# A fused attention and two-layer kernel on one core: second group of early weights loaded behind chunk 22, attention rows of chunks 16 to 23 stored after chunk 23

## The chip, the cores and the metric

The kernel runs on one core of one Trainium2 chip. The metric is the device time in microseconds (us) of one execution. Three runs of the kernel before gave 1062.04, 1062.69 and 1062.05 us; the median is 1062.05 us. The profiled execution took 1062.24 us, with a span of 1060.5 us from its first to its last instruction, so 1.7 us lie around the span.

## The reference, cut to what matters

```
# decayed linear attention, 4 batches, 8 heads, 768 positions, head size 64
for t in range(S):
    state = gamma[None, :, None, None] * state + np.einsum('bhd,bhe->bhde', k[:, :, t], v[:, :, t])
    y[:, :, t] = scale * np.einsum('bhd,bhde->bhe', q[:, :, t], state)
x = y.transpose(0, 2, 1, 3).reshape(3072, 512)
# first layer (512 -> 2048 -> 512)
h = np.maximum(x @ w_in, 0.0); x = h * h @ w_out
# second layer (512 -> 1536 -> 512), gated, behind an RMS norm
xn = x / sqrt(mean(x * x) + 1e-06) * rms_g
out = (silu(xn @ w_gate) * (xn @ w_val)) @ w_out2
```

## The kernel before, in words

**Stages.** The kernel is written engine by engine, with explicit semaphores; every engine runs its own list in order. First comes the attention, in 24 chunks of 128 positions (4 batches of 6 chunks). Then come two layers over three token tiles. Every 2x2 block matrix product in them is done with seven block products (a Strassen form), and every factor is split into a high and a low part, so that a product is three matmuls (lines 898 to 900).

**Attention.** The q, k and v rows of a chunk (1 MiB, or 0.75 MiB for the last chunk of a batch) go into one of five places of `qkv_sb`. SyncE's list issues the load of chunk n+5 when chunk n is done (line 473). TensorE does, for a chunk, the scores (line 820, one chunk ahead), the part from the state (line 839), the state's update (line 873) and the masked part (line 849). VectorE masks the scores (line 1389), scales the state (line 1398) and copies the chunk's result out (line 1378). Eight results go straight into `raw`, where the first token tile is made. The other 16 go to DRAM (`x_scratch`), issued from ScalarE's list by `store_x` (line 1003), through three small places of `y_sb` in turn. The results of chunks 18 to 23 are held: those of 18 to 22 are issued in ScalarE's round for chunk 22, and that of 23 in the round for chunk 23. The held results of chunks 21 to 23 lie in freed parts of `qkv_sb`.

**Early weights.** During the attention GpSimd and ScalarE also prepare two groups ("quads") of the first layer's second weights. A quad is 1 MiB and is loaded in two halves (`load_early_quad`, line 486) into the place that `raw_w[:, 0]` or `[:, 1]` leaves. It is made into seven items: 11 units, of which four are sums (lines 769 to 779) and seven are the low parts of the items (line 785), in the order of units 0 to 10. ScalarE casts the high part of each item first (`high_quad`, line 1068). The 14 items lie in `spare` (items 0 to 3), in the second operands of `ops` (items 4 to 11) and in the place of chunk 19 in `qkv_sb` (items 12 and 13). SyncE then stores each to DRAM (`store_item`, line 498). Quad 1 keeps its sums in `sums_w[:, 2]` and `[:, 3]`. In the kernel before, quad 1 is loaded behind the loads of chunks 16 and 17.

**First product run.** The first run of the first layer (run 0) has seven products, k = 0 to 6, of 12 matmuls each. Its operands k = 3 to 6 lie in the places of `ops` that the early items have used. So ScalarE's cast of operand k (`high_front`, line 1046) waits until the items in its place have landed in DRAM: items 4 and 5 for k=3, 6 and 7 for k=4, 8 and 9 for k=5, 10 and 11 for k=6. VectorE makes the low part of each (`low_front`, line 1404). TensorE's k=2 waits for `seed(0)`, a copy from bank X to bank Y by ScalarE (line 1099), and its k=6 waits for `c22_done`, an addition by VectorE (line 1692). On VectorE's list stand, between the low parts of k=4 and k=5, three sums of run 1's weights (`sum_w`, lines 1538 to 1543), which write `sums_w`.

Of the kernel before, what the change touches and what calls it, by code (L numbers as in the profile page):

```python
# [18 lines left out]
CH = S // P  # L19
# [22 lines left out]
FIRST = 3  # L42
HELD = NCH - 6
LAST_FREED = (NCH - RING) % RING
# [97 lines left out]
def build(nc, qkv, decay_rows, tables, identity, w_f1, w_f2, w_b, rms_g, out):  # L142
# [6 lines left out]
    with ExitStack() as ctx:  # L149
# [40 lines left out]
        y_copied = sem("y_copied")  # L190
        x_stored = [sem(f"x_stored{i}") for i in range(3)]

# [213 lines left out]

        EARLY = [(0, u) for u in range(9)] + [(1, 0), (1, 1), (0, 9), (0, 10)] + [(1, u) for u in range(2, 11)]

        def early_at(x):
            return 10 + x * 14 // 22  # L410

        def early_casts(n):

            at, found = 0, []
            for x, (quad, u) in enumerate(EARLY):
                if unit_item(u) is not None:
                    at = max(at, early_at(x) - (2 if ITEMS[unit_item(u)] in SUMMED else 3))
                    if 7 * quad + unit_item(u) >= EARLY_PLACES - 2:
                        at = max(at, NCH - RING + 1)
                    if at == n:  # L420
                        found.append((quad, unit_item(u)))
            return found

# [15 lines left out]
        def stored_y(n):  # L439

            if n >= HELD + 3:
                return (qkv_sb[:, 0, V, :], qkv_sb[:, 1, V, :], qkv_sb[:, 2, QT, :])[n - HELD - 3]
            return y_sb[:, stored_chunks().index(divmod(n, CH)) % 3, :]

        def x_place(b, c):
# [17 lines left out]
        def _(sp):  # L463
# [44 lines left out]
            for n in range(NCH - RING):  # L508
                sp.wait_ge(chunk_done, n + 1)
                if n % CH == 0:  # L510
                    sp.wait_ge(state_done, updates_by(n))
                load_chunk(n + RING)
                if n == 1:
                    load_raw_w(0)
                if n in (4, 6):
                    load_early_quad(0, (n - 4) // 2)
                if n == 8:
                    sp.dma_start(gains[:], rms_g).then_inc(consts_loaded, 16)
                if n in (11, 12):
                    sp.wait_ge(w_lo, 7)  # L520
                    load_early_quad(1, n - 11)
            for i in (4, 5):
                store_item(0, i)
            sp.wait_ge(quad_lo, 7)
            load_raw_w(1)
            for i in (6, 7, 8, 9, 10, 11, 0, 1, 2, 3, 12, 13):
                store_item(*divmod(i, 7))
# [33 lines left out]
            def front_free(front):  # L561

                sp.wait_ge(front_lo, 7 * front)
                if front == 1:
                    for i in range(5):
                        sp.wait_ge(kept3[i], 16 * len(range(i, 7, 5)))
                sp.wait_ge(quad_lo, 7 * min(3 + front, QUADS))
                if front < TILES:
                    for i in range(3):
                        sp.wait_ge(x_stored[i], 16 * len(stored_chunks()[i::3]))  # L570

# [423 lines left out]
        def _(act):  # L995
            def store_x(n):

                b, c = divmod(n, CH)
                if (b, c) not in stored_chunks():
                    return  # L1000
                i = stored_chunks().index((b, c))
                act.wait_ge(y_copied, n + 1)
                act.dma_start(x_dram[i].rearrange("p h k t -> p (h k t)"), stored_y(n))\
                    .then_inc(x_stored[i % 3], 16)

# [162 lines left out]
            def first_run():  # L1168

                seed(0)  # L1170
                high_front(0, 3)
                high_front(0, 4)
                save_p5(0)
                save_u2(0)
                high_w(1, 0)
                high_front(0, 5)
                high_front(0, 6)
# [7 lines left out]
            def front_run(run, m, fresh, front, bk=None):  # L1185
# [15 lines left out]
                if m == 1:  # L1201
                    for i in range(3):
                        act.wait_ge(x_stored[i], 16 * len(stored_chunks()[i::3]))
                tail(run - 1)
# [126 lines left out]
            for n in range(NCH):  # L1331
# [10 lines left out]
                if n < HELD:  # L1342
                    store_x(n)
                elif n == NCH - 2:
                    for held in range(HELD, NCH - 1):
                        store_x(held)
                elif n == NCH - 1:
                    store_x(n)
            for t in range(TILES):
# [15 lines left out]
        def _(dve):  # L1365
            def copy_out(n):
# [6 lines left out]
                else:  # L1373
                    i = stored_chunks().index((b, c))
                    if 3 <= i and n < HELD + 3:
                        dve.wait_ge(x_stored[i % 3], 16 * (i // 3))
                    place = stored_y(n).rearrange("p (a b t) -> p a b t", a=2, b=2)
# [152 lines left out]
            def sum_w(m, i):  # L1530

                A11, A12, A21, A22 = (raw_w[:, m % 2, a] for a in range(4))
                if i == 0:
                    dve.wait_ge(raw_w_loaded[m % 2], 16 * (m // 2 + 1))
                    dve.wait_ge(w_lo, 7 * m - 1)
                    if m == 1:
                        dve.wait_ge(quad_lo, 14)
                    op = nc.vector.tensor_tensor(sums_w[:, 0], A21, A22, ALU.add)
                elif i == 1:
# [9 lines left out]
            def quad_unit(quad, unit):  # L1549

                A11, A12, A21, A22 = (quad_raw(quad, a) for a in range(4))
                if unit in (0, 1, 4, 8):
                    if unit == 0:
                        if quad == 2:
                            for i in range(3):
                                dve.wait_ge(x_stored[i], 16 * len(stored_chunks()[i::3]))
                        dve.wait_ge(quad_lo, 7 * quad)
# [397 lines left out]
```

## Time and profile before

| | |
|---|---|
| median of three runs | 1062.05 us |
| profiled execution | 1062.24 us |
| its span | 1060.5 us |
| TensorE busy | 1050.8 us (99%) |
| VectorE busy | 882.0 us (83%) |
| ScalarE busy | 609.2 us (57%) |
| GpSimd busy | 331.8 us (31%) |
| granted TensorE clock | 1.00 |

The granted clock was full over the whole span. The busy shares are means over stages; the change lies in the attention and in the first run behind it, which together are the first tenth of the span.

### The profile page before, as it was taken

How to read it: one execution, taken by the hardware profiler on the slowest of the kernel's cores; microseconds unless marked ns; L12 is line 12 of the kernel's file. 1: busy time of each engine (PE TensorE's matmuls, PEld its weight loads, DVE VectorE, ACT ScalarE, POOL GpSimd, SP SyncE). 2: the span in 40 equal slices, each digit the busy share in tenths (PEclk: the TensorE clock that was granted, in tenths of full speed). 3: DMA queues.
4: the chain of work that ended last, by engine and by line, in shares of the span. 5: the costliest groups of instructions: out<-in, count | busy, mean ns of one | idle time of the engine just before them, and what ended most of it. 6: DMA issues, size and time to landing. Idle time of an engine off the chain costs nothing.

```text
span 1060.5 us, 15146 instructions
## 1 busy us (share of the span) xinstructions
PE 1050.8 (99%) x5742; PEld 870.1 (82%) x5742; DVE 882.0 (83%) x935; ACT 609.2 (57%) x879; POOL 331.8 (31%) x244
## 2 busy tenths in 40 slices
PE   8989999999999999999999999999999999999999
PEld 6878888888888888888888888888888888888887
DVE  5887989879779878789899988978886986978696
ACT  4875765557664666654674645556445555544453
POOL 1864550005530015430034554005444102544000
DMA  9999568654438644365642335632225751140456
GB/s 365 414 419 417 206 230 267 214 191 139 179 126 273 216 144 156 139 258 195 221 146 96 119 120 219 217 120 81 60 65 154 261 194 60 46 117 21 138 192 186
DMA packets 82759, 195.74 MB, mean 185 GB/s; under 512 B 30584, under 2 KB 39416, under 8 KB 75648
## 3 DMA queue, kind: packets, MB, share of 16 engines
q1 hardware_dynamic: 76960, 189.74, 51.4%
q10 hardware_dynamic: 5728, 5.04, 1.4%
q8 instruction: 46, 0.75, 0.3%
q14 instruction: 25, 0.20, 0.1%
HBM read 152.17 MB, written 42.48 MB: 184 GB/s over the span
## 4 chain that ended last, share of the span: by engine, by line
PE 96%; DMA 3%; SPq 0%; issue 0%; ACT 0%
PE Y L898 13%; PE Y L900 13%; PE Y L899 13%; PE X L898 9%; PE Z L898 9%; PE Z L900 9%; PE X L899 9%; PE Z L899 9%; PE X L900 9%; DMA qkv_sb<-qkv 3%; PE Z L849 1%; PE X L820 1%; PE Y L820 1%; PE R L873 1%; PE Z L839 1%; PE R L849 0%
## 5 line engine op out<-in xcount | busy, mean ns | idle before, releaser
L743 POOL TENSOR_TENSOR w_ops<-raw_w,w_ops 128x512 fp32r<-128x512 f32 x90 | 127.9, 1421 | 497.1 <-ACT w_ops L1027 497.0
L1091 ACT CAST ops<-hid 128x1024 fp32r<-128x1024 f32 x147 | 154.6, 1054 | 155.6 <-PE Y L900 53.3
L1492 DVE TENSOR_TENSOR ops<-hid,ops 128x1024 fp32r<-128x1024 f32 x147 | 179.9, 1226 | 37.9 <-ACT ops L1091 37.4
L743 POOL TENSOR_TENSOR w_ops<-sums_w,w_ops 128x512 fp32r<-128x512 f32 x120 | 167.4, 1398 | 120.9 <-ACT w_ops L1027 120.3
L898 PE MATMUL Y<-ops,w_ops 128*128 128x512 f32 x360 | 140.1, 389 | 0.0
L900 PE MATMUL Y<-ops,w_ops 128*128 128x512 f32 x360 | 140.1, 389 | 0.0
L899 PE MATMUL Y<-ops,w_ops 128*128 128x512 f32 x360 | 140.1, 389 | 0.0
L1116 ACT ACTIVATE gt<-gt 128x512 f32<-128x512 f32 x72 | 45.1, 633 | 111.7 <-DVE gt L1712 38.9
L898 PE MATMUL Y<-ops 128*128 128x512 f32 (+1 forms) x264 | 100.3, 380 | 0.0
L899 PE MATMUL Y<-ops 128*128 128x512 f32 (+1 forms) x264 | 100.1, 379 | 0.0
L900 PE MATMUL Y<-ops 128*128 128x512 f32 (+1 forms) x264 | 100.1, 379 | 0.0
L1027 ACT CAST w_ops<-sums_w 128x512 fp32r<-128x512 f32 x120 | 74.2, 621 | 39.5 <-PE Y L900 16.7
L898 PE MATMUL X<-ops,w_ops 128*128 128x512 f32 x240 | 93.5, 389 | 0.0
L900 PE MATMUL Z<-ops,w_ops 128*128 128x512 f32 x240 | 93.4, 389 | 0.0
L899 PE MATMUL X<-ops,w_ops 128*128 128x512 f32 x240 | 93.4, 389 | 0.0
L900 PE MATMUL X<-ops,w_ops 128*128 128x512 f32 x240 | 93.4, 389 | 0.0
L898 PE MATMUL Z<-ops,w_ops 128*128 128x512 f32 x240 | 93.4, 389 | 0.0
L899 PE MATMUL Z<-ops,w_ops 128*128 128x512 f32 x240 | 93.4, 389 | 0.0
L898 PEld LDWEIGHTS Y<-ops,w_ops 128*128 128x128 f32 x360 | 67.6, 188 | 14.2
L900 PEld LDWEIGHTS Y<-ops,w_ops 128*128 128x128 f32 x360 | 67.6, 188 | 14.1
L1404 DVE TENSOR_TENSOR ops<-raw,ops 128x1024 fp32r<-128x1024 f32 x39 | 55.7, 1435 | 28.1 <-ACT ops L1046 28.1
L899 PEld LDWEIGHTS Y<-ops,w_ops 128*128 128x128 f32 x360 | 67.6, 188 | 14.0
(182 smaller groups left out, 2249.4 us busy)
## 6 DMA issues: line engine op xcount, KB each, us to landing
ops<-item_scratch SPq DMA_DIRECT2D x147, 512.0 KB, 3.4
raw_w<-w_f SPq DMA_DIRECT2D x30, 1024.0 KB, 5.2
qkv_sb<-qkv SPq DMA_DIRECT2D x17, 1024.0 KB, 9.6
item_scratch<-hid SPq DMA_DIRECT2D x30, 512.0 KB, 3.3
y_scratch<-hid SPq DMA_DIRECT2D x12, 512.0 KB, 5.8
raw<-y_scratch SPq DMA_DIRECT2D x3, 2048.0 KB, 9.6
raw<-w_b SPq DMA_DIRECT2D x5, 1024.0 KB, 4.9
out<-hid SPq DMA_DIRECT2D x36, 128.0 KB, 5.3
```

The costliest lines, as they stand in the source:

```text
L743: nc.gpsimd.tensor_tensor(w_ops[:, k, 1], front_w_source(m, k), f32(w_ops[:, k, 0]), ALU.subtract).then_inc(w_lo, 1)
L820: mm = nc.tensor.matmul(scores_ps[n % 2][:, h % 2, cols], qkv_sb[rows, n % RING, KT, cols], qkv_sb[rows, n % RING, QT, cols], start=h < 2, ...
L839: nc.tensor.matmul(y_place(n, h), state[rows, c % 2, p, :], qkv_sb[rows, n % RING, QT, P * p:P * p + P], start=p < 2, stop=False, skip_gro ...
L849: mm = nc.tensor.matmul(y_place(n, h), qkv_sb[:, n % RING, V, h * D:(h + 1) * D], masked[:, c % 2, h % 2, P * p:P * p + P], start=c == 0 a ...
L898: nc.tensor.matmul(dst, left_hi, right_hi, start=start, stop=False, skip_group_check=True)
L899: nc.tensor.matmul(dst, left_hi, right_lo, start=False, stop=False, skip_group_check=True)
L900: return nc.tensor.matmul(dst, left_lo, right_hi, start=False, stop=True, skip_group_check=True)
L1027: nc.scalar.copy(w_ops[:, k, 0], front_w_source(m, k)).then_inc(w_hi, 1)
L1091: nc.scalar.copy(hop_at(bk, n)[:, 0], hid[:, 2 * g:2 * g + 2, OPERAND[k], :])\
L1116: nc.scalar.activation(gt[:, i % 2, :], gt[:, i % 2, :], ACT.Silu).then_inc(gate_out, 1)
L1404: nc.vector.tensor_tensor(front_lo_at(k), raw_slot(OPERAND[k]), f32(front_hi_at(k)), ALU.subtract).then_inc(front_lo, 1)
L1492: nc.vector.tensor_tensor(hop[:, 1], hid[:, 2 * g:2 * g + 2, OPERAND[k], :], f32(hop[:, 0]), ALU.subtract).then_inc(own_lo if bk.own_place ...
```

## The change

The two loads of quad 1 move from behind chunks 16 and 17 to behind chunk 22. The list of units (`EARLY`) is now in plain order, so that quad 0 is finished before quad 1 begins; ScalarE's casts of quad 1's items 0 to 5 stand in its rounds for chunks 20 to 22, and that of item 6 in run 0. The stores of the results of chunks 16 and 17 are held too, and all eight held stores stand in ScalarE's round for chunk 23. The results of chunks 16 and 17 wait in `sums_w[:, 0]` and `[:, 1]`, so there are a fourth `x_stored` semaphore and new waits on VectorE: `copy_out` of chunks 16 and 17 waits for quad 0's items, and the first `sum_w` of run 1's weights waits until those two results have landed in DRAM. SyncE stores item 0 (from `spare`) second.

```
-HELD = NCH - 6
+HELD = NCH - 8
+IN_SLOTS = NCH - 3
...
-        EARLY = [(0, u) for u in range(9)] + [(1, 0), (1, 1), (0, 9), (0, 10)] + [(1, u) for u in range(2, 11)]
+        EARLY = [(quad, u) for quad in range(2) for u in range(11)]
...
-            return 10 + x * 14 // 22
+            return 10 + x * 14 // 22 if x < 11 else 21 + (x - 11) // 4
...
-            return found
+            return found + [(1, i) for i, late in enumerate((20, 21, 21, 21, 22, 22)) if late == n]
...
+            if n in (HELD, HELD + 1):
+                return sums_w[:, n - HELD].rearrange("p k d -> p (k d)")
...
+        def stores_on(j):
+
+            in_sums = [stored_chunks().index(divmod(n, CH)) for n in (HELD, HELD + 1)]
+            if j == 3:
+                return in_sums
+            return [i for i in range(j, len(stored_chunks()), 3) if i not in in_sums]
...
-                if n in (11, 12):
+                if n == NCH - RING - 2:
                     sp.wait_ge(w_lo, 7)
-                    load_early_quad(1, n - 11)
+                    load_early_quad(1, 0)
+                    load_early_quad(1, 1)
...
-            for i in (6, 7, 8, 9, 10, 11, 0, 1, 2, 3, 12, 13):
+            for i in (6, 0, 7, 8, 9, 10, 11, 1, 2, 3, 12, 13):
                 store_item(*divmod(i, 7))
...
                 seed(0)
                 high_front(0, 3)
+                high_quad(1, 6)
+                save_p5(0)
                 high_front(0, 4)
-                save_p5(0)
                 save_u2(0)
+                high_front(0, 5)
                 high_w(1, 0)
-                high_front(0, 5)
                 high_front(0, 6)
...
-                elif n == NCH - 2:
-                    for held in range(HELD, NCH - 1):
+                elif n == NCH - 1:
+                    for held in range(HELD, NCH):
                         store_x(held)
-                elif n == NCH - 1:
-                    store_x(n)
...
+                    if n in (HELD, HELD + 1):
+                        dve.wait_ge(quad_lo, 7)
+                    elif 3 <= i and n < IN_SLOTS:
+                        dve.wait_ge(x_stored[i % 3], 16 * len([j for j in stores_on(i % 3) if j < i]))
...
                     if m == 1:
                         dve.wait_ge(quad_lo, 14)
+                        dve.wait_ge(x_stored[3], 32)
```

SyncE's list of DMAs between the load of chunk 15 and run 0, before (`raw_w<-w_b` is a half of quad 1, `qkv_sb<-qkv` a chunk, `item_scratch` an item's store, `raw_w<-w_f` run weights; 128x1536 is a last chunk of a batch):

```order
L486 DMA raw_w<-w_b 128x1024 [waits w_lo]
L473 DMA qkv_sb<-qkv 128x2048 [waits chunk_done] x5
L473 DMA qkv_sb<-qkv 128x1536 [waits state_done,chunk_done]
L498 DMA item_scratch<-ops 128x1024 [waits quad_lo] x2
L480 DMA raw_w<-w_f 128x2048 [waits quad_lo]
L498 DMA item_scratch<-ops 128x1024 [waits quad_lo] x6
```

and now:

```order
L485 DMA qkv_sb<-qkv 128x2048 [waits chunk_done] x5
L498 DMA raw_w<-w_b 128x1024 [waits w_lo]
L498 DMA raw_w<-w_b 128x1024
L485 DMA qkv_sb<-qkv 128x1536 [waits state_done,chunk_done]
L510 DMA item_scratch<-ops 128x1024 [waits quad_lo] x2
L492 DMA raw_w<-w_f 128x2048 [waits quad_lo]
L510 DMA item_scratch<-ops 128x1024 [waits quad_lo]
L510 DMA item_scratch<-spare 128x1024 [waits quad_lo]
```

Both halves of quad 1 now stand between chunk 22 (the last of the five) and chunk 23; before, the second half stood ahead of chunks 18 to 22.

ScalarE's list from its last chunk scaling (`k_dec`) to the second wait for landed items, before:

```order
L1068 CAST qkv_sb<-raw_w 128x512 [waits quad_loaded0,chunk_done]
L1068 CAST qkv_sb<-sums_w 128x512 [waits quad_sum,chunk_done]
L1003 DMA x_scratch<-y_sb 128x512 [waits y_copied] x3
L1003 DMA x_scratch<-qkv_sb 128x512 [waits y_copied] x3
L1099 COPY Y<-X 128x1024 [waits product_done]
L1046 CAST ops<-raw 128x1024 [waits early_kept5,early_kept4]
L1046 CAST ops<-raw 128x1024 [waits front_t,early_kept7,early_kept6]
L1105 COPY p<-Z 128x1024 [waits product_done]
```

and now:

```order
L1081 CAST ops<-raw_w 128x512 [waits quad_loaded0]
L1081 CAST ops<-sums_w 128x512 [waits quad_sum]
L1081 CAST ops<-raw_w 128x512 [waits quad_loaded0]
L1081 CAST ops<-sums_w 128x512 [waits quad_sum] x2
L1081 CAST qkv_sb<-raw_w 128x512 [waits quad_loaded0,chunk_done]
L1016 DMA x_scratch<-sums_w 128x512 [waits y_copied] x2
L1016 DMA x_scratch<-y_sb 128x512 [waits y_copied] x3
L1016 DMA x_scratch<-qkv_sb 128x512 [waits y_copied] x3
L1112 COPY Y<-X 128x1024 [waits product_done]
L1059 CAST ops<-raw 128x1024 [waits early_kept5,early_kept4]
L1081 CAST qkv_sb<-sums_w 128x512 [waits quad_sum,chunk_done]
L1118 COPY p<-Z 128x1024 [waits product_done]
```

Six casts of quad 1 and eight store issues now stand directly ahead of the copy Y<-X, which is `seed(0)`, and the cast of item 6 stands behind the operand k=3.

## Rows read from the trace of the kernel before

**Rows 1.** The page, part 4: the chain that ended last, by engine.
```profile
PE 96%; DMA 3%; SPq 0%; issue 0%; ACT 0%
```

**Rows 2.** Windows: busy us (x instructions) of PE, PEld, DVE, ACT, POOL; clock, DMA, GB/s.
```profile
63.00:78.00 15.00, 13.35 (x255) 11.44 (x256) 12.88 (x20) 12.28 (x43) 10.71 (x9) 1.00 1.02 418
78.00:94.00 16.00, 16.00 (x182) 13.22 (x175) 10.69 (x16) 6.60 (x11) 4.01 (x3) 1.00 1.03 414
```

**Rows 3.** The chain in order of time (start us, us, what), the load of chunk 21.
```profile
62.17 11.11 DMA qkv_sb<-qkv
```

**Rows 4.** Timeline of TensorE: start us, us, instruction, count, [idle before it, and its releaser].
```profile
63.02 1.16 PE L820 MATMUL X<-qkv_sb 64*128 64x128 f32 x16 [0.90 <-DMA qkv_sb<-qkv]
...
66.11 1.16 PE L820 MATMUL Y<-qkv_sb 64*128 64x128 f32 x16 [0.30 <-DMA qkv_sb<-qkv]
...
69.20 1.16 PE L820 MATMUL X<-qkv_sb 64*128 64x128 f32 x16 [0.44 <-DMA qkv_sb<-qkv]
...
73.33 1.16 PE L820 MATMUL Y<-qkv_sb 64*128 64x128 f32 x16 [0.88 <-DMA qkv_sb<-qkv]
...
79.69 1.16 PE L820 MATMUL Y<-qkv_sb 64*128 64x128 f32 x16
...
90.06 0.39 PE L898 MATMUL Y<-ops,w_ops 128*128 128x512 f32 x1
...
100.94 0.39 PE L898 MATMUL Y<-ops,w_ops 128*128 128x512 f32 x1
```

**Rows 5.** One line's DMAs in a window, from issue to landing: quad 1's second half.
```profile
L486 SPq DMA_DIRECT2D raw_w<-w_b x1: 647/647/647, 49.5 to 49.5; - x1
...
DMA to landing us min/median/max: 10.5/10.5/10.5
```

**Rows 6.** The same for the loads of chunk 22 and of chunk 23.
```profile
L473 SPq DMA_DIRECT2D qkv_sb<-qkv x1: 328/328/328, 65.8 to 65.8; - x1
...
DMA to landing us min/median/max: 10.2/10.2/10.2
...
L473 SPq DMA_DIRECT2D qkv_sb<-qkv x1: 327/327/327, 68.8 to 68.8; - x1
...
DMA to landing us min/median/max: 9.0/9.0/9.0
```

**Rows 7.** Timeline of GpSimd: quad 1's unit 0 and unit 3.
```profile
60.11 1.28 POOL L769 TENSOR_TENSOR sums_w<-raw_w 128x512 f32<-128x512 f32 x1 [5.64 <-DMA raw_w<-w_b]
...
63.81 1.73 POOL L785 TENSOR_TENSOR ops<-sums_w,ops 128x512 fp32r<-128x512 f32 x1
```

**Rows 8.** Timeline of ScalarE: the six held stores, and seed(0).
```profile
79.17 1.60 ACTq L1003 DMA_DIRECT2D x_scratch<-y_sb  x3
80.81 4.85 ACTq L1003 DMA_DIRECT2D x_scratch<-qkv_sb  x3
87.54 1.00 ACT L1099 COPY Y<-X 128x1024 f32<-128x1024 f32 x1 [7.78 <-PE X L900]
```

**Rows 9.** Timeline of VectorE: the first sum of run 1's weights, and c22.
```profile
92.95 0.69 DVE L1538 TENSOR_TENSOR sums_w<-raw_w 128x512 f32<-128x512 f32 x1
...
99.39 1.21 DVE L1692 TENSOR_TENSOR hid<-Y,p 128x1024 f32<-128x1024 f32 x1
```

**Rows 10.** From issue to landing: the held stores, all six (min/median/max).
```profile
L1003 ACTq DMA_DIRECT2D x_scratch<-y_sb x3: 326/586/609, 79.2 to 80.2; - x3
L1003 ACTq DMA_DIRECT2D x_scratch<-qkv_sb x3: 326/327/631, 80.8 to 85.3; - x3
...
DMA to landing us min/median/max: 7.5/10.1/11.2
```

**Rows 11.** The same for the store of item 11.
```profile
L498 SPq DMA_DIRECT2D item_scratch<-ops x1: 319/319/319, 77.2 to 77.2; - x1
...
DMA to landing us min/median/max: 16.7/16.7/16.7
```

More of the change, by code:

```diff
@@ L190, in build @@
         y_copied = sem("y_copied")
-        x_stored = [sem(f"x_stored{i}") for i in range(3)]
+        x_stored = [sem(f"x_stored{i}") for i in range(4)]
         consts_loaded = sem("consts_loaded")
@@ L405, in tokens @@
             return ps[:].rearrange("p z n -> p (z n)").rearrange("p (t d) -> p t d", t=4)
-        EARLY = [(0, u) for u in range(9)] + [(1, 0), (1, 1), (0, 9), (0, 10)] + [(1, u) for u in range(2, 11)]
+        EARLY = [(quad, u) for quad in range(2) for u in range(11)]
         def early_at(x):
-            return 10 + x * 14 // 22
+            return 10 + x * 14 // 22 if x < 11 else 21 + (x - 11) // 4
         def early_casts(n):
             at, found = 0, []
-            for x, (quad, u) in enumerate(EARLY):
+            for x, (quad, u) in enumerate(EARLY[:11]):
                 if unit_item(u) is not None:
                     at = max(at, early_at(x) - (2 if ITEMS[unit_item(u)] in SUMMED else 3))
-                    if 7 * quad + unit_item(u) >= EARLY_PLACES - 2:
-                        at = max(at, NCH - RING + 1)
                     if at == n:
                         found.append((quad, unit_item(u)))
-            return found
+            return found + [(1, i) for i, late in enumerate((20, 21, 21, 21, 22, 22)) if late == n]
         def unit_item(unit):
@@ L439, in stored_y, with store_sem @@
         def stored_y(n):
-            if n >= HELD + 3:
-                return (qkv_sb[:, 0, V, :], qkv_sb[:, 1, V, :], qkv_sb[:, 2, QT, :])[n - HELD - 3]
+            if n >= IN_SLOTS:
+                return (qkv_sb[:, 0, V, :], qkv_sb[:, 1, V, :], qkv_sb[:, 2, QT, :])[n - IN_SLOTS]
+            if n in (HELD, HELD + 1):
+                return sums_w[:, n - HELD].rearrange("p k d -> p (k d)")
             return y_sb[:, stored_chunks().index(divmod(n, CH)) % 3, :]
+        def stores_on(j):
[3 more added lines that the diff above has]
+            return [i for i in range(j, len(stored_chunks()), 3) if i not in in_sums]
+        def store_sem(i):
+            return next(j for j in range(4) if i in stores_on(j))
         def x_place(b, c):
@@ L568, in front_free @@
                 if front < TILES:
-                    for i in range(3):
-                        sp.wait_ge(x_stored[i], 16 * len(stored_chunks()[i::3]))
+                    for i in range(4):
+                        sp.wait_ge(x_stored[i], 16 * len(stores_on(i)))
             def load_front(front):
@@ L1003, in store_x @@
                 act.dma_start(x_dram[i].rearrange("p h k t -> p (h k t)"), stored_y(n))\
-                    .then_inc(x_stored[i % 3], 16)
+                    .then_inc(x_stored[store_sem(i)], 16)
             def scale_k(n):
@@ L1201, in front_run @@
                 if m == 1:
-                    for i in range(3):
-                        act.wait_ge(x_stored[i], 16 * len(stored_chunks()[i::3]))
+                    for i in range(4):
+                        act.wait_ge(x_stored[i], 16 * len(stores_on(i)))
                 tail(run - 1)
@@ L1374, in copy_out @@
                     i = stored_chunks().index((b, c))
-                    if 3 <= i and n < HELD + 3:
-                        dve.wait_ge(x_stored[i % 3], 16 * (i // 3))
+                    if n in (HELD, HELD + 1):
+                        dve.wait_ge(quad_lo, 7)
+                    elif 3 <= i and n < IN_SLOTS:
+                        dve.wait_ge(x_stored[i % 3], 16 * len([j for j in stores_on(i % 3) if j < i]))
                     place = stored_y(n).rearrange("p (a b t) -> p a b t", a=2, b=2)
@@ L1554, in quad_unit @@
                         if quad == 2:
-                            for i in range(3):
-                                dve.wait_ge(x_stored[i], 16 * len(stored_chunks()[i::3]))
+                            for i in range(4):
+                                dve.wait_ge(x_stored[i], 16 * len(stores_on(i)))
                         dve.wait_ge(quad_lo, 7 * quad)
```

## The prediction, written before the changed kernel ran

> **What bounds the kernel now.** I read the chain that ended last first: 96% of the span is TensorE and 3% is loads of chunk rows [rows 1]. So a change pays only where TensorE waits, and later work can only be shifted. The timeline of TensorE shows where it waits near the change. Four times, before the scores of chunks 18 to 21, it stands idle for a chunk's rows: 0.90, 0.30, 0.44 and 0.88 us, together 2.52 us [rows 4]. Behind 73.33 it has no idle time. The chain says the same: the load of chunk 21 is issued at 62.17 and lands 11.11 us later, at 73.3 [rows 3]. The windows show why a load takes so long: from 63 to 94 us the DMA engines are full, at 414 to 418 GB/s [rows 2]. At 418 GB/s 1 MiB costs 2.5 us and a result of 0.25 MiB 0.6 us.
>
> Run 0 begins without a wait, but two of its products hang on other engines. Product k=2 starts at 90.06 and k=6 at 100.94, 10.88 us later [rows 4]. VectorE's c22, which k=6 waits for, ends at 99.39+1.21 = 100.60 [rows 9]. So only 0.34 us lie between that addition and a wait, and this is the place to watch.
>
> **Part 1: quad 1's 1 MiB leaves the way of chunks 18 to 22, and two results leave it too.** Quad 1's second half, issued at 49.5, landed at 60.0 [rows 5], ahead of chunk 18. Without the quad each of the following loads lands 2.5 us earlier for the same issue time. The largest single wait is 0.90 us, and since the waits add up (a load is issued when a chunk is done, so an earlier chunk also issues earlier), the need moves by at most 2.52 us. All four waits then go. What is late next is VectorE: it was busy 12.88 of 15 us from 63 to 78 [rows 2], so in the 12.5 us that are left of this stretch it has no idle time. I keep back 0.2 us for it (0 to 0.5). Gain of this part: 2.3 us (2.0 to 2.5).
>
> **Part 2: does chunk 23 come in time?** It now stands behind quad 1, but the bytes ahead of it are the same ones as before, less two results. It landed at 68.8+9.0 = 77.8 [rows 6], so it now lands at 77.8-1.2 = 76.6 (77.4 if only one of the two results was ahead of it). TensorE began its scores at 79.69 [rows 4] and will now want them at 77.2 to 77.4. Cost 0, at most 0.2.
>
> **Part 3: quad 1 is late.** Chunk 22 landed at 65.8+10.2 = 76.0 [rows 6]. Less 2.5 for the quad and 0.6 to 1.2 for results it lands at 72.3 to 72.9, and the quad behind it 2.5 us later, near 75.1 (74.8 to 75.4); before it was there at 60.0. GpSimd needs units 0 to 4 before ScalarE can cast item 4: four of 1.28 us and one of 1.28 to 1.73 [rows 7], 6.6 us, so 81.7. ScalarE casts items 4 and 5 and comes to the eight stores at about 82.4. All eight results are copied by then but that of chunk 23, which comes at about 83, in time for its place at the end of the list.
>
> Eight issues: the first three took 1.60 us, and single ones 0.33 to 0.63 us [rows 8, 10]. That is 2.6 to 5.0 us; I take 3.9, as the middle, since those of about 0.6 fell while SyncE was issuing too, and now SyncE's item stores are spread out. Seed(0) then starts at 86.3 (85.3 to 87.9). Product 0 is ready for it at 87.54-2.3 = 85.2 [rows 8]. Its end, 87.3, is ahead of k=2's new place at 90.06-2.3 = 87.8. So the seed itself costs nothing in the middle case.
>
> **Part 4: the chain from the seed to c22.** Behind the seed ScalarE has operand k=3, item 6, the copy of Z and operand k=4: 1.0, 1.0, 0.5, 1.0 and 1.0 us with the seed (by the 1.00 of a copy of 128x1024 [rows 8], a cast of half a size taken as 0.5). Then VectorE has, one behind the other, the low part of k=4, three sums at 0.69 (0.67 apart) [rows 9], the low parts of k=5 and k=6, the product with X and c22, each of the last at 1.15 to 1.21 us [rows 9]. That is 4.5 + 1.2 + 2.0 + 3x1.15 + 1.2 = 12.35, and 0.1 for semaphores: k=6 can start 12.5 us behind the seed's start, at 98.8. Its free place is 100.94-2.3 = 98.6. Cost 0.2 (0 to 1.8); from a seed at 86.1 on, every microsecond of it costs one.
>
> **Part 5: the place of operand k=6 is free later.** Item 11 was issued at 77.2 and landed at 93.9 [rows 11]. Between chunk 23's landing at 77.8 and that, 5 MiB of SyncE's went over (run 1's weights and eight items of 0.5 MiB), and about 1.4 of ScalarE's (five results landed, and a part of the sixth). Now item 0 is added, 5.5 MiB, and the results start 3 us later: with the same share of about 1.4 they make 6.9 MiB at 0.397 MiB per us (6.4 MiB in 16.1 us), 17.4 us from 76.6: 94.0. Operand 6, its low part, X and c22 behind it take 1.0 + 1.2 + 1.15 + 1.2 + 0.2 = 4.75, so k=6 at 98.8. Hidden beside part 4, with nothing to spare. The results' share rests on rows 10: first landing at 86.7 and the last, issued at 85.3, near 95.4, so one per 1.8 us.
>
> The Trainium skill ("DMA: Bandwidth & Descriptors", section "Queues, rings and completion order") says that each DMA engine goes round robin between the queue rows that have work, a packet at a time. Taken as equal halves, ScalarE's queue would get all its 2 MiB through ahead of item 11, and k=6 would start at 76.6 + 7.5/0.397 + 4.75 = 100.2, a gain of 0.7 us. The trace speaks for a smaller share: one result per 1.8 us is 0.14 of 0.397 MiB per us, a little over a third [rows 2, 10].
>
> **Sum.** 2.3 - 0.2 - 0.1 (for parts 4 and 5 meeting) = 2.0 us at k=6 of run 0. Behind it the same work stands: only the weights of run 2 are now loaded behind 0.5 MiB more of results (1.3 us) and are wanted 2 us earlier, by VectorE's sums in run 1. No row here prices that; I take 0.1 for it, and 0 to 1 as its bounds. The span goes from 1060.5 to 1058.6, the profiled execution from 1062.24 to 1060.3, and the median, which stands 0.2 us under that execution, from 1062.05 to 1060.2.
>
> **Rivals.** A measurement of this kernel tells 0.2%, 2.1 us, from no change.
>
> *A. Nothing takes the waits' place.* The eight issues take about 3 us (0.33 to 0.4 each [rows 10]), the seed starts by 86.0, and all of the 2.2 to 2.5 us stay: 1059.5 to 1059.9. For it: the issues of 0.6 us had SyncE beside them. Against: three margins of under 0.3 us have to hold at once.
>
> *B. ScalarE's stores, or item 11, hold run 0 back.* At 0.63 us an issue the seed starts at 87.4 and k=6 at 99.9: gain 1.0. Equal shares of the queues give 0.7. With both, or with a quad that lands 1 us later, the gain is 0 to 0.5: 1061.5 to 1062. For it: issues of 0.6 us are in the rows [rows 10].
>
> *C. Slower: VectorE waits for the results in `sums_w`.* The first sum of run 1's weights now waits until the results of chunks 16 and 17 have landed. They are issued at about 82.4 and 82.8, and everything of part 4 on VectorE stands behind that wait: k=6 starts 2.0 + 3x1.15 + 1.2 + 0.1 = 6.75 us behind the landing. With the 7.5 us of the fastest held store that is 90.3, before the 92.0 at which VectorE comes there: cost 0. With the median of 10.1 it is 92.9 and the gain 1.3; with the 11.2 of the slowest [rows 10] it is 94.0 and all but 0.2 of the gain is lost. From a latency of 11.4 us it is slower than before, and from 13.5 by over 0.2%. SyncE's item store took 16.7 us in the same full queues [rows 11]; at that price k=6 starts at 106.2 or so and the time is 1067.3. Against it: no store of ScalarE's took over 11.2, and these two are the first of theirs.
>
> *D. The change does not speed up the attention.* If VectorE or chunk 23 is as late as the rows were, the loads were not the limit: gain 0.5 at most, 1061.6.
>
> **How the numbers follow.** Forecast (gain 1.2 to 2.1, centre 1.9): 0.38. A: 0.34. B, where the gain is under 1.2: 0.12. C: 0.12, of which 0.08 with a loss of over 0.2%. D: 0.04. The forecast, B, D and the rest of C lie within 0.2%. So faster by over 0.2% is A, 0.34; within 0.2% is 0.38 + 0.12 + 0.04 + 0.04 = 0.58; slower is 0.08. The predicted time is 1060.2. The range from 1059.5 to 1062.8 leaves out the slower part of C (0.08) and a gain over 2.5 us (a few in a hundred).
>
> **What the changed profile would show.** TensorE's idle time before scores of chunks 18 to 21 gone, and its first product at 82.2 (84.5 before). The load of quad 1 landing near 75. GpSimd waiting from about 59 to 75. The first held store issued near 82.4 and seed(0) at 86.3. A wait of TensorE before k=2 of run 0 would say that the stores were dearer; one before k=6 with VectorE idle ahead of a sum would be C, with ScalarE idle ahead of operand 6 it would be part 5. If TensorE has over 0.5 us of idle before the scores of chunks 18 to 23, part 1 or 2 is wrong.

## The result and the profile after

The changed kernel takes 1066.55 us, median of six runs (1065.63 to 1067.79), against 1062.1 us of the kernel before (1061.86 to 1063.52). The ratio is 1.004, with a 95% interval from 1.0028 to 1.0051: slower by about 4.4 us. The forecast was 1060.2 us with a range to 1062.8, so its sign and its range were wrong. The profiled execution took 1066.84 us, its span is 1065.0 us (1060.5 before).

First the timeline of TensorE in the changed kernel, the scores of chunks 18 and 21 and each place where it waits up to product k=6 of run 0 (start us, us, instruction, [idle before it, and its releaser]):

```profile
62.03 1.16 PE L833 MATMUL X<-qkv_sb 64*128 64x128 f32 x16
...
68.69 0.67 PE L852 MATMUL Z<-qkv_sb,state 64*64 64x128 f32 x16 [0.20 <-DVE state L1412]
70.78 1.16 PE L833 MATMUL Y<-qkv_sb 64*128 64x128 f32 x16
...
81.10 0.67 PE L852 MATMUL R<-qkv_sb,state 64*64 64x128 f32 x16 [0.72 <-DVE state L1412]
...
82.72 0.50 PE L911 MATMUL X<-ops,w_ops 128*128 128x512 f32 x1
...
90.39 0.50 PE L911 MATMUL Y<-ops,w_ops 128*128 128x512 f32 x1 [1.93 <-ACT Y L1112]
...
101.20 0.47 PE L911 MATMUL Z<-ops,w_ops 128*128 128x512 f32 x1 [2.12 <-DVE ops L1418]
...
105.60 0.50 PE L911 MATMUL Y<-ops,w_ops 128*128 128x512 f32 x1 [1.40 <-DVE hid L1707]
```

The four waits for chunk rows [rows 4] are gone; two small waits for VectorE stand in their place. Run 0 begins at 82.72. But k=2 starts at 90.39 (90.06 before), and k=6 at 105.60 (100.94 before): 4.66 us late. The span is 4.5 us longer, so the whole loss has come about by then, and 0.2 us of it is made good later. Behind k=6 the trace has no more waits of TensorE.

ScalarE's timeline, in the stretch that answers to [rows 8]: the last two casts ahead of the stores, the stores (ACTq), seed(0) and what follows it.

```profile
82.10 0.62 ACT L1081 CAST ops<-sums_w 128x512 fp32r<-128x512 f32 x1 [3.72 <-POOL sums_w L788]
82.19 1.27 ACTq L1016 DMA_DIRECT2D x_scratch<-sums_w  x2
82.63 0.61 ACT L1081 CAST qkv_sb<-raw_w 128x512 fp32r<-128x512 f32 x1
83.51 2.25 ACTq L1016 DMA_DIRECT2D x_scratch<-y_sb  x3
85.80 3.50 ACTq L1016 DMA_DIRECT2D x_scratch<-qkv_sb  x3
89.34 1.00 ACT L1112 COPY Y<-X 128x1024 f32<-128x1024 f32 x1 [6.09 <-PE Z L913]
90.25 1.05 ACT L1059 CAST ops<-raw 128x1024 fp32r<-128x1024 f32 x1
```

The eight issues take from 82.19 to 89.30, 7.1 us. The seed's releaser is given as TensorE, with 6.09 us of idle time, but the last matmul of product 0, which the seed waits for, ended at 85.8 (85.36 + 0.39); the semaphore came early and the list itself was busy with the issues. The chain of waits says so: it goes through the issues one by one.

```profile
84.58 1.18 ACTq L1016
...
85.80 1.11 ACTq L1016
...
88.14 1.16 ACTq L1016
```

VectorE's timeline behind the seed, from the low part of k=3 to c22, which answers to [rows 9]:

```profile
91.33 1.23 DVE L1418 TENSOR_TENSOR ops<-raw,ops 128x1024 fp32r<-128x1024 f32 x1 [7.80 <-ACT ops L1059]
92.47 2.32 DVE L1460 TENSOR_TENSOR raw<-raw 128x1024 f32<-128x1024 f32 x1
94.72 1.21 DVE L1418 TENSOR_TENSOR ops<-raw,ops 128x1024 fp32r<-128x1024 f32 x1
95.85 0.68 DVE L1553 TENSOR_TENSOR sums_w<-raw_w 128x512 f32<-128x512 f32 x1
96.56 1.68 DVE L1558 TENSOR_TENSOR sums_w<-sums_w,raw_w 128x512 f32<-128x512 f32 x1
...
98.77 4.51 DVE L1418 TENSOR_TENSOR ops<-raw,ops 128x1024 fp32r<-128x1024 f32 x2
103.20 1.21 DVE L1703 TENSOR_TENSOR hid<-hid,X 128x1024 f32<-128x1024 f32 x1
104.33 1.21 DVE L1707 TENSOR_TENSOR hid<-Y,p 128x1024 f32<-128x1024 f32 x1
```

VectorE never rests from 91.33 on, and some instructions take 1.0 to 1.1 us more than their like: the combination 2.32 (1.22 before), a sum 1.68 (0.69 before), the two low parts 4.51 together (2.84 before). GpSimd's timeline shows what ran beside them:

```profile
91.89 1.81 POOL L798 TENSOR_TENSOR qkv_sb<-sums_w,qkv_sb 128x512 fp32r<-128x512 f32 x1 [2.96 <-ACT qkv_sb L1081]
96.14 1.56 POOL L756 TENSOR_TENSOR w_ops<-raw_w,w_ops 128x512 fp32r<-128x512 f32 x1 [2.43 <-ACT w_ops L1040]
98.52 3.69 POOL L756 TENSOR_TENSOR w_ops<-sums_w,w_ops 128x512 fp32r<-128x512 f32 x2 [0.82 <-ACT w_ops L1040]
102.16 2.27 POOL L756 TENSOR_TENSOR w_ops<-raw_w,w_ops 128x512 fp32r<-128x512 f32 x1
```

The same places in the kernel before, VectorE's combination and its two low parts, and GpSimd's first low parts of run 1's weights:

```profile
90.68 1.22 DVE L1446 TENSOR_TENSOR raw<-raw 128x1024 f32<-128x1024 f32 x1
...
95.50 2.84 DVE L1404 TENSOR_TENSOR ops<-raw,ops 128x1024 fp32r<-128x1024 f32 x2 [0.53 <-ACT ops L1046]
```

```profile
94.59 1.53 POOL L743 TENSOR_TENSOR w_ops<-raw_w,w_ops 128x512 fp32r<-128x512 f32 x1 [12.35 <-ACT w_ops L1027]
97.92 2.83 POOL L743 TENSOR_TENSOR w_ops<-sums_w,w_ops 128x512 fp32r<-128x512 f32 x2 [1.79 <-ACT w_ops L1027]
```

The last unit of quad 1 runs at 91.89; before it ran at 80.53, and GpSimd then idled for 12.35 us beside this chain. Of GpSimd's low parts of run 1's weights, the second and third began before at 97.92, when VectorE was nearly through with its pair; now they begin at 98.52, beside both low parts of the operands.

The lengths follow a pattern. A two-input instruction of VectorE on SBUF operands that begins while one of GpSimd's runs is longer by what was left of GpSimd's, less about 0.1 us. The combination began at 92.47, GpSimd's unit ended at 93.70: 1.23 us left, 1.10 longer. The first low part of the pair before began at 95.50 and GpSimd's ended at 96.12: 0.62 left, and the pair was 0.5 longer than in x1_gap, where GpSimd starts nothing ahead of it. When VectorE's begins first it keeps its length and GpSimd's is the longer one: 1.23 us for the low part at 91.33, and 1.81 in place of 1.27 for the unit at 91.89. So the two take turns, and what counts is which of them is running when the other begins.

### The profile page after: what moved, and what is told of

The parts are those of the page before. It is cut to its first block, busy times and chain, and to the rows that moved or that the text cites. A ratio compares the mean times of both kernels' runs of the same rounds, so it can differ in the third digit from the quotient of the medians.

```text
span 1065.0 us, 15149 instructions
## 1 busy us (share of the span) xinstructions
PE 1051.6 (99%) x5742; PEld 870.0 (82%) x5742; DVE 883.3 (83%) x935; ACT 609.1 (57%) x879; POOL 333.0 (31%) x244
## 4 chain that ended last, share of the span: by engine, by line
PE 94%; DMA 3%; DVE 2%; issue 1%; ACTq 1%; SPq 0%; ACT 0%; DVEq 0%
PE Y L911 13%; PE Y L912 13%; PE Y L913 13%; PE Z L912 9%; PE X L912 9%; PE Z L911 9%; PE X L911 9%; PE Z L913 9%; PE X L913 9%; DMA qkv_sb<-qkv 2%; PE Z L862 1%; DMA x_scratch<-y_sb 1%; PE X L833 1%; PE R L886 1%; PE Z L852 1%
## 5 line engine op out<-in xcount | busy, mean ns | idle before, releaser
L911 PE MATMUL Z<-ops,w_ops 128*128 128x512 f32 x240 | 93.5, 389 | 2.1 <-DVE ops L1418 2.1
L911 PE MATMUL X<-ops,w_ops 128*128 128x512 f32 x240 | 93.5, 390 | 0.0
```

The lines of the kernel that those rows point to most:

```text
L911: nc.tensor.matmul(dst, left_hi, right_hi, start=start, stop=False, skip_group_check=True)
```

## The experiments

Two theories stood beside each other. S: the stores ahead of the seed make the loss. G: GpSimd beside VectorE stretches the chain behind the seed. In the table, "run 0" is TensorE's first product, "seed" the start of seed(0), "k=6" the start of that product; times of the profiled execution, and the median, with the ratio to the kernel before measured beside it.

| kernel | run 0 | seed | k=6 | span | median, ratio (95%) |
|---|---|---|---|---|---|
| before | 84.49 | 87.54 | 100.94 | 1060.5 | 1062.1 |
| changed | 82.72 | 89.34 | 105.60 | 1065.0 | 1066.55, 1.004 (1.0028 to 1.0051) |
| x1_gap | 83.19 | 86.25 | 101.38 | 1060.8 | 1062.55, 0.9997 (0.9986 to 1.0009) |
| x3_sp_quiet | 81.57 | 87.08 | 101.29 | 1060.6 | 1062.52, one run |
| x4_held6 | 82.82 | 86.95 | 104.20 | 1063.7 | 1065.5, 1.003 (1.0019 to 1.004) |
| x7_dve_units | 83.26 | 89.77 | 104.01 | 1063.4 | 1065.11, 1.0028 (1.0019 to 1.0037) |
| x6_gap_dve | 84.06 | 88.08 | 101.21 | 1060.5 | 1061.87, 0.9995 (0.9986 to 1.0004) |
| x10_gap_order | 81.89 | 84.94 | 101.19 | 1060.5 | 1062.39, 1.0 (0.9991 to 1.0009) |
| x9_best | 83.28 | 87.30 | 99.75, no wait | 1059.8 | 1060.82, 0.9987 (0.9978 to 0.9996) |

In every kernel of the table but the last the span is the start of k=6 plus 959.3 to 959.6 us: that product is where the difference is decided. In x9_best it is 960.0 us, so 0.5 us of its gain is lost again later. The start of run 0 scatters from execution to execution: x3_sp_quiet differs from the changed kernel only in what comes later, and starts it at 81.57 in place of 82.72. A difference of about 1 us in that column is not read as the work of an edit.

**x1_gap: six of the stores in ScalarE's idle time.**

```
-                elif n == NCH - 1:
-                    for held in range(HELD, NCH):
-                        store_x(held)
+                elif n == NCH - 3:
+                    for held in range(HELD, NCH - 2):
+                        store_x(held)
+                elif n == NCH - 1:
+                    for held in range(NCH - 2, NCH):
+                        store_x(held)
```

> The changed kernel, with the stores of the held results of chunks 16 to 21 issued at the end of ScalarE's round for chunk 21, where it is idle for 3.7 us (78.4 to 82.1), and only those of chunks 22 and 23 left ahead of seed(0). Theory S (the eight store issues ahead of the seed delay k=2, k=5 and k=6 of run 0): seed(0) starts at 85.9 to 86.5 in place of 89.3, TensorE's wait before k=2 (1.9 us) is gone, and k=6 starts about 3 us earlier, near 102.6; the time is 1063.5 to 1064. Rival G (the chain behind the seed is stretched by GpSimd working beside VectorE, and keeps its length of 16.2 us or grows, since GpSimd's units of quad 1 are not earlier): k=6 is earlier by less than 2 us, the time over 1064.5. Rival Q (the issues are dear wherever they stand, 1.1 us each behind the fourth, so the fifth cast and all behind it shift by 2 us): seed at 87 to 88.

The seed came at 86.25, TensorE's wait before k=2 was gone, and k=6 came 4.2 us earlier, more than S said; the time is that of the kernel before, below the 1063.5 that S allowed. G as the only cause and Q are out. The stores' place alone takes the whole loss away, though part of it was G's: with an earlier seed the two low parts of k=5 and k=6 ran ahead of GpSimd's low parts (2.35 us together, 4.51 in the changed kernel), while the low part of k=3 and the combination now met the last units of quad 1:

```profile
88.25 2.26 DVE L1421 TENSOR_TENSOR ops<-raw,ops 128x1024 fp32r<-128x1024 f32 x1 [4.25 <-ACT ops L1059]
90.43 2.31 DVE L1463 TENSOR_TENSOR raw<-raw 128x1024 f32<-128x1024 f32 x1
...
96.71 2.35 DVE L1421 TENSOR_TENSOR ops<-raw,ops 128x1024 fp32r<-128x1024 f32 x2
```

**x3_sp_quiet: no stores of SyncE beside ScalarE's.** Ahead of item 9 SyncE waits for the seed (`if i == 9: sp.wait_ge(seeded, 1)`).

> The changed kernel, with SyncE's item stores from item 9 on held until seed(0) is done, so that SyncE issues no DMA while ScalarE issues its eight stores. If the issues are dear because SyncE issues at the same time: 0.33 to 0.5 us each, eight in under 4 us, seed(0) near 86.3. If they are dear because more than four stores of ScalarE's own queue are outstanding: still 1.1 us each from the fifth on, seed(0) near 89. Items 9 to 11 land later in either case, so the time itself may be above that of the changed kernel.

The eight issues took 5.0 us (82.05 to 87.03) and the seed came at 87.08: between the two forecasts, nearer to the first. DMA issues and time from issue to landing of the last six and all eight, here and in the changed kernel:

```profile
L1018 ACTq DMA_DIRECT2D x_scratch<-y_sb x3: 474/523/526, 83.5 to 84.6; - x3
L1018 ACTq DMA_DIRECT2D x_scratch<-qkv_sb x3: 542/627/642, 85.1 to 86.4; - x3
...
DMA to landing us min/median/max: 3.8/5.2/5.5
```

```profile
L1016 ACTq DMA_DIRECT2D x_scratch<-y_sb x3: 492/500/1176, 83.5 to 84.6; - x3
L1016 ACTq DMA_DIRECT2D x_scratch<-qkv_sb x3: 1115/1152/1156, 85.8 to 88.1; - x3
...
DMA to landing us min/median/max: 4.0/8.7/11.5
```

0.47 to 0.64 us for each of the last six here, against 1.1 to 1.2 for the last four there: with SyncE's stores held back, eight issues in a row are cheaper, so their number alone does not set the price. Two things changed at once, SyncE's issuing at the same time and the fuller queues (a landing within 5.5 us here, 11.5 there). Other traces speak against the first as the whole cause. In x10_gap_order three issues in a row, from 79.40 to 82.45, took 0.93 to 1.10 us each, while SyncE issued two stores of 0.32 us each, and landings took 8.3 to 11.1 us. In the kernel before, two issues at 83.71 and 85.33 took 0.33 us each beside issues of SyncE of 1.7 to 2.0 us; each stood over 1 us behind ScalarE's previous one. What the dear issues have in common is a row of them without a pause, into queues with long landings; a run that changes only one of the two is missing. Items 9 to 11 came later, and still the time was 4 us under the changed kernel.

**x4_held6: six held stores in place of eight** (`HELD = NCH - 6` in the changed kernel).

> The changed kernel with HELD back at NCH - 6: the results of chunks 16 and 17 are stored when they are made, six stores stand in ScalarE's round for chunk 23, and the results of chunks 18 and 19 lie in sums_w. Theory S: two issues less at 1.15 us, so seed(0) at 87 in place of 89.3, and k=6 2 us or more earlier than 105.6, the time 1063.5 to 1065. In the attention the two stores are back between the loads of chunks 22 and 23: chunk 23 lands 1.2 us later and run 0 starts at 83 to 83.8 in place of 82.8. Rival (the stores' number is not what counts, only GpSimd beside VectorE): seed earlier, but k=6 at 105 or later and the time at 1066 or more.

Seed at 86.95, as expected, but k=6 only 1.4 us earlier. The low part of k=3, the combination and a sum took 2.10, 2.31 and 1.77 us and the two last low parts 4.51: the time that the seed gave was taken by GpSimd. The time, 1065.5 us, lies between both forecasts. Chunk 23 came later, as expected: TensorE waited 0.93 us for its rows. Here both theories were half right: the number of stores sets the seed, and what GpSimd does then decides how much of it arrives.

**x7_dve_units: VectorE makes quad 1's units 5 to 10.** GpSimd stops at unit 4, VectorE does the rest at 84 to 90, and the cast of item 6 stands ahead of the seed.

```
-                for x, (quad, unit) in enumerate(EARLY):
+                for x, (quad, unit) in enumerate(EARLY[:16]):
...
+            dve.wait_ge(quad_sum, 7)
+            dve.wait_ge(quad_lo, 9)
+            for unit in range(5, 11):
+                quad_unit(1, unit)
```

> The changed kernel with VectorE making quad 1's units 5 to 10, and the cast of item 6 ahead of the seed, but all eight stores still ahead of the seed. Theory S: the seed stays at 89 to 90 and TensorE's wait before k=2 stays near 2 us (2.5 with the cast). Theory G: the third combination goes from 2.3 to 1.2 us and k=6 starts 1 to 2 us earlier than 105.6, the time is 1064.5 to 1066. If GpSimd's units were the whole of it: 1063 or less.

As G said: the low part of k=3 took 1.23 and the combination 1.22 us, the seed and TensorE's wait before k=2 (1.83 us) stayed, and k=6 came 1.6 us earlier than in the changed kernel. So of the two causes, taken alone, the stores' place is worth 4.2 us at k=6 and the units 1.6; by the medians, against the changed kernel's, 4.0 and 1.4.

**x8_pool_dummy: GpSimd's work added to the kernel before.** Three subtractions, a wait for `front_hi` ahead of them, nothing else.

```
+            pool.wait_ge(quad_lo, 14)
+            pool.wait_ge(front_hi, 4)
+            for j in range(3):
+                if j:
+                    pool.wait_ge(scratched, j)
+                nc.gpsimd.tensor_tensor(sums_w[:, 3], f32(w_ops[:, 6, 0]), f32(w_ops[:, 6, 1]), ALU.subtract)\
+                    .then_inc(scratched, 1)
```

> The kernel before, with three subtractions of 128x512 added on GpSimd, which begin when ScalarE has cast operand k=3 (89.5); they read weights at rest and write sums_w[3], which nobody else uses until VectorE's fourth sum (100.5), and nothing else changes. Theory G (GpSimd's work stretches VectorE's two-input work on the same memory): of VectorE's low part of k=3, third combination, low part of k=4 and three sums, which took 1.22 and 0.69 us each, two or three take 1 us longer, c22 ends 2 to 3 us later than 100.6, less the 0.5 us that VectorE was idle, and the time grows by 1 to 2.5 us. Rival (the stretch in the changed kernel came from the DMA traffic or from ScalarE): no change in VectorE's times, and the time stays at 1062 to 1062.7.

1068.9 us against 1062.21, ratio 1.0065 (1.0053 to 1.0078). VectorE's and GpSimd's timelines:

```profile
91.16 2.31 DVE L1454 TENSOR_TENSOR raw<-raw 128x1024 f32<-128x1024 f32 x1
93.39 2.32 DVE L1412 TENSOR_TENSOR ops<-raw,ops 128x1024 fp32r<-128x1024 f32 x1
95.63 1.78 DVE L1546 TENSOR_TENSOR sums_w<-raw_w 128x512 f32<-128x512 f32 x1
97.45 1.67 DVE L1551 TENSOR_TENSOR sums_w<-sums_w,raw_w 128x512 f32<-128x512 f32 x1
...
100.72 4.50 DVE L1412 TENSOR_TENSOR ops<-raw,ops 128x1024 fp32r<-128x1024 f32 x2
```

```profile
90.12 6.74 POOL L812 TENSOR_TENSOR sums_w<-w_ops 128x512 f32<-128x512 f32 x3 [7.39 <-ACT ops L1054]
```

G is shown, and more strongly than expected: every instruction of VectorE in this list, each begun while one of GpSimd's ran, took about 1.1 us more (1.22 to 2.31, 0.69 to 1.67 or 1.78), and GpSimd's own took 2.2 in place of 1.3, each waiting for the other in turn. The low part of k=3, begun at 90.02 ahead of the first dummy at 90.12, kept its 1.22. The expectation was too low because the delay feeds itself: VectorE, late by the dummies, then met all of the low parts that it had missed before. c22 ended 6.9 us late. TensorE's clock fell in this run too (the last section), but k=6 started 0.07 us behind the end of c22, so VectorE set the time. The Trainium skill has the rule that counts here ("GPSIMD Engine Reference", section "Specifications"): GpSimd shares its interfaces to SBUF with VectorE, which collides with VectorE's instructions that have two inputs in SBUF. The trace agrees: up to 1.1 us for a VectorE instruction that begins beside a GpSimd one of 1.3; the products with X and with Y, which have one input in PSUM, kept their 1.21 us beside GpSimd in the changed kernel (103.20 and 104.33, beside 102.16).

**x2_w_late: GpSimd's weights behind c22.** The casts k=1 to 4 of run 1's weights stand behind `raise_d`.

> The changed kernel, with ScalarE's casts k=1 to 4 of run 1's weights put behind the two activations of raise_d in the first run, so that GpSimd has no low part of weights to make while VectorE makes the low parts of operands k=5 and k=6 and the two products behind them. Theory G (GpSimd's work stretches VectorE's): the two low parts, which took 4.51 us together, take 2.4 to 2.8, k=6 starts near 103.6 in place of 105.6, and the time is 1064.3 to 1065, unless run 1 then waits for its weights. Rival S (only the store issues delay the run): the two low parts still take over 4 us, and the time is 1066.5 or more.

A miss. k=6 came at 103.68, as G said, but the two low parts still took 3.46 us, since GpSimd's first low part (97.73) met one of them, and run 1 waited 2.7 us for what hangs on the late weights: 1069.85 us, ratio 1.006 (1.0037 to 1.0083). GpSimd's work can't just be put off.

**x5_early_loads: quad 1 loaded where it was** (behind chunks 16 and 17), with the changed kernel's casts and stores.

> The changed kernel, with the two loads of quad 1 put back behind the loads of chunks 16 and 17; the order of units and casts and the eight held stores stay. If the gain of the attention comes from the loads' place: TensorE waits again before the scores of chunks 18 to 21, about 2 us in all, and run 0 starts at 84 to 84.5 in place of 82.8. GpSimd's first sums are done by 63, but the casts still stand in rounds 20 to 22, so the fifth cast no longer waits for unit 4 (82.1) and comes at 79 to 80; the eight issues then start near 80 and seed(0) at 86 to 87.5. Theory S: k=6 starts at 101.5 to 103, the time is 1062.5 to 1064. Rival (the order of the list behind the seed costs by itself): still above 1065.

1067.48 us, ratio 1.0039 (1.0026 to 1.0052). TensorE's waits for chunk rows were back, 1.38 and 0.27 us before the scores of two chunks, and run 0 started at 84.11, 1.4 us later than in the changed kernel. The waits show that the attention's gain comes from the loads' place; by the scatter of that start, its size is known to about 1 us. The rest of the expectation was wrong: the fifth cast still came at 82.08, since unit 4 stands behind items whose casts wait for their rounds, and the seed at 90.27. The time is above 1065, as the rival said, but by the late seed: from the seed to k=6 (106.54) it takes 16.3 us, as in the changed kernel. Nothing of the loss comes from the loads as such.

**x6_gap_dve, x9_best, x10_gap_order: the two remedies together.** x6_gap_dve has both edits of x1_gap and x7_dve_units.

> The changed kernel with the stores of chunks 16 to 21 in ScalarE's gap (as in x1_gap), and besides VectorE in place of GpSimd makes quad 1's units 5 to 10, in its own gap between the last copy of the attention and the low part of operand k=3 (83.5 to 88 in x1_gap), with the cast of item 6 ahead of seed(0). Theory S+G (the stores ahead of the seed, and GpSimd's units beside VectorE's, are the whole loss): the low part of k=3 and the third combination take 1.2 us each (2.3 with GpSimd beside them), c22 ends by 99.5, TensorE has no wait behind its start at 83.2, and the span is 1059.2 to 1059.6, 1.0 to 1.3 us under the kernel before. Rival (landing of items 10 and 11 is the next limit): ScalarE idle ahead of operand k=6 until 95.5, c22 at 100.2 to 100.8, the time that of the kernel before within 0.5 us.

The rival was nearer. The low part of k=3 and the combination took 1.23 and 1.22 us, but operand k=6 was cast only at 96.07, behind 1.05 us of idle time of ScalarE, and the two last low parts took 3.45 us beside a low part of GpSimd at 95.10. So the last two kernels add:

```
-            for i in (6, 0, 7, 8, 9, 10, 11, 1, 2, 3, 12, 13):
+            for i in (6, 7, 8, 9, 10, 11, 0, 1, 2, 3, 12, 13):
...
                 high_front(0, 5)
-                high_w(1, 0)
                 high_front(0, 6)
+                high_w(1, 0)
```

> The kernel of x6_gap_dve with two more changes of order: item 0 is stored behind item 11 again, and ScalarE casts operand k=6 ahead of the first of run 1's weights. Theory: what limits x6_gap_dve behind the seed is the landing of item 11 (ScalarE idle 1.05 us ahead of operand k=6, cast at 96.07) and GpSimd's low part at 95.1 beside VectorE's two low parts (3.45 us). Then operand 6 is cast by 95, the two low parts take 2.3 to 2.5 us, c22 ends by 100.1, TensorE has no wait behind the attention, and the time is what the attention gained, 1061.0 to 1061.7. Rival (nothing behind the seed limits any more, the attention's own waits do): the same time as x6_gap_dve within 0.3 us.

> The kernel of x1_gap (GpSimd makes all of quad 1) with the same two changes of order as x9_best. Theory G: GpSimd's last two units still stretch the low part of k=3 and the third combination to 2.3 us each, so c22 ends 0.5 to 1.5 us later than in x9_best and the time is 0.3 to 1.2 us above it. Rival (the item's landing was the only limit): the time equals that of x9_best.

x9_best takes 1060.82 us against 1062.42, ratio 0.9987 (0.9978 to 0.9996): a gain of 1.6 us, small but clear of no change. Operand 6, the two low parts and c22 (ended at 99.70) came as expected. x10_gap_order stands 1.57 us above it, c22 1.4 us later: theory G, by more than the 1.2 us of its time forecast; x9_best's rival and x10_gap_order's are both out. ScalarE's operands 5 and 6 and VectorE's pair in x9_best, and VectorE's first three and the pair in x10_gap_order:

```profile
92.68 1.05 ACT L1059 CAST ops<-raw 128x1024 fp32r<-128x1024 f32 x1
94.81 1.05 ACT L1059 CAST ops<-raw 128x1024 fp32r<-128x1024 f32 x1 [1.08 <-issue]
```

```profile
94.66 2.47 DVE L1421 TENSOR_TENSOR ops<-raw,ops 128x1024 fp32r<-128x1024 f32 x2
```

```profile
86.94 2.15 DVE L1421 TENSOR_TENSOR ops<-raw,ops 128x1024 fp32r<-128x1024 f32 x1 [4.25 <-ACT ops L1059]
89.02 2.31 DVE L1463 TENSOR_TENSOR raw<-raw 128x1024 f32<-128x1024 f32 x1
91.25 2.32 DVE L1421 TENSOR_TENSOR ops<-raw,ops 128x1024 fp32r<-128x1024 f32 x1
...
95.42 3.45 DVE L1421 TENSOR_TENSOR ops<-raw,ops 128x1024 fp32r<-128x1024 f32 x2
```

TensorE has no wait before any product of run 0 in x9_best. In these runs the attention's gain arrives only with all three: the stores in the gap, quad 1's last units off GpSimd (x10_gap_order lacks that, starts run 0 earlier still, at 81.89, and loses all of it before k=6), and the two changes of order (x6_gap_dve lacks those).

## Why the prediction was wrong

- **Part 1, the loads leave the way: right, mis-sized.** All four waits went. The 0.2 us kept back for VectorE was 0.92 (0.20 and 0.72 us before the state products), so run 0 started at 82.72 and not 82.2. The larger of the two stands behind VectorE's half low part at 77.86 in the chain of waits, 1.66 us long (0.70 before), beside GpSimd's units of quad 1, which are now there: the cause of part 4's failure, already at work in the attention. x3_sp_quiet and x10_gap_order, at 81.57 and 81.89, show that the whole 2.5 us can be had.
- **Part 2, chunk 23: right.** No wait for it.
- **Part 3, quad 1 is late: right up to the stores, then the step that failed first.** GpSimd's first sum came at 75.05 (75.1 said), the first store at 82.19 (82.4). But eight issues took 7.1 us and not 3.9, outside the bounds of 2.6 to 5.0. These were taken from issues at 0.33 to 0.63 us [rows 8, 10], of which no more than four stood in a row; now there were eight, at 0.9 us in the mean and 1.1 to 1.2 from the fifth on. The reading that the dear ones of before were those beside SyncE's issues was wrong as well: two of the three at 0.33 us (83.71 and 85.33) stood beside them too. The seed came 3.0 us late.
- **Part 4, the chain from the seed to k=6: the step that failed worst.** 16.3 us and not 12.5: 0.9 more up to VectorE's low part of k=4 (the combination ahead of it, which stands in no term of the sum, was stretched and came last), 0.9 more for the sums, 2.1 more for the two low parts. Every duration in it came from a moment at which GpSimd was idle; the sum treated GpSimd only as a supplier of quad 1. The trace of before had the warning: two low parts at 2.84 us together beside GpSimd, where single ones took 1.22; that they ran beside GpSimd was not asked. x8_pool_dummy shows the mechanism, x7_dve_units its price here.
- **Part 5, item 11: right.** It landed at 93.5 (94.0 said), with the share of the queues taken from the rows; by the rival of equal shares it would have been 95.5 (76.6 + 7.5/0.397).
- **Rival C, the slower one: wrong mechanism.** The stores of chunks 16 and 17 landed 4.0 and 5.7 us after issue, long before VectorE came to the sum at 95.85. The kernel got slower by what was booked as terms of the sum, not by the new wait. B named the dearer issues, and stopped at 0.63 us each.

The balance at k=6: 1.77 us gained in the attention, 2.10 lost before k=2 (the seed), 2.65 before k=5 and 1.68 before k=6 (VectorE behind a late seed, and stretched): 4.66 us in all.

## What to carry to other kernels

Work that is moved off the busy transfer queue lands on other engines at another time, so ask for each of its instructions what runs beside it there, above all for GpSimd and VectorE on SBUF operands: here VectorE waited out the rest of GpSimd's instruction, up to 1.1 us each time. DMA issues in an engine's list are work of that engine, and many in a row belong where it is idle, not ahead of the operation that releases TensorE. A slack of 0.3 us before the bounding engine is the first thing to protect.

## What the runs showed of the hardware that was not expected

An issue of a 256 KB store from ScalarE cost 0.33 us as the first of a row or behind a pause of over 1 us, and 1.1 to 1.2 us from the fifth of an unbroken row on, with landings of up to 11.5 us. What of this sets the price is open, as x3_sp_quiet says. The Trainium skill ("DMA: Bandwidth & Descriptors", section "Issuing engines are not separate DMA queues") calls the issuing time usually small beside the transfer. For a single store the trace agrees, 1.2 us at most against 4.0 to 11.5 us to its landing; but eight took 7.1 us of ScalarE's list, on the path that sets the end.

A wait of TensorE can slow the matmuls behind it. In x2_w_late it was idle for 2.1 us ahead of k=2 (90.52), and the granted clock fell behind that wait. Windows of that kernel: start:end, sum, busy us of PE, PEld, DVE, ACT and POOL with counts, then granted clock, DMA share and GB/s.

```profile
88.00:90.00 2.00, 0.40 (x2) 0.00 (x0) 0.00 (x0) 0.53 (x1) 0.87 (x1) 1.00 1.04 416
90.00:92.00 2.00, 1.48 (x6) 1.20 (x7) 0.53 (x1) 2.00 (x4) 0.00 (x0) 0.90 1.03 414
92.00:94.00 2.00, 2.00 (x6) 1.59 (x5) 2.00 (x2) 1.81 (x2) 1.81 (x1) 0.50 1.04 415
94.00:96.00 2.00, 2.00 (x8) 1.55 (x7) 2.00 (x3) 0.83 (x1) 0.00 (x0) 0.75 1.04 415
```

0.50 is the lower of its two levels, 1.2 GHz: in the two microseconds from 92 to 94 six matmuls went through in place of eleven, and product k=2 took 4.4 us in place of 2.85. x5_early_loads and x8_pool_dummy show the same 0.50 from 104 to 106, behind waits of 2.16 and 4.28 us before k=5. In none of the three did it cost time at k=6: VectorE worked without a pause from the low part of k=3 to c22, and the starts of k=6 (103.68, 106.54, 107.55) stand within 0.1 us of c22's end. Nor does a wait of 2 us always bring it: the profiled execution of the changed kernel kept the full clock behind waits of 1.93 and 2.12 us. Four of its other five runs show a mean of 0.998, as x2_w_late's profile does, so they may have met it, but their times (1065.63 to 1067.79 us) are not above those of the two at 1.00 (1066.84 and 1067.04) as a group: the clock does not explain the loss.
